# Gated attention and two FFNs: the first FFN's weight pieces through five staging buffers, high and low halves in slots of their own

## The reference

```python
state = f[:, :, t, :, None] * state + np.einsum('bhd,bhe->bhde', k[:, :, t], v[:, :, t])   # f = sigmoid(f_logit)
y[:, :, t] = np.einsum('bhd,bhde->bhe', q[:, :, t], state)
```

## Time and profile before

| | us |
|---|---|
| median of 3 runs (1322.17 to 1323.76) | 1322.76 |
| the profiled execution, its own time | 1321.92 |
| span of the profiled execution | 1320.1 |
| PE busy | 1306.3 |
| DVE (VectorE) busy | 832.0 |
| ACT busy | 623.1 |
| POOL (GpSimd) busy | 548.4 |
| PE's granted clock | 1.00 in every slice |

### The profile page before, as it was taken

How to read it: one execution, slowest core, us unless ns; L and a number is a source line. 1 busy time by engine, 2 the same in 40 slices (tenths; PEclk the granted TensorE clock), 3 DMA queues, 4 the chain that set the end, 5 groups by cost and what they waited for, 6 DMA issues and landing times.

```text
span 1320.1 us, 23658 instructions
## 1 busy us (share of the span) xinstructions
PE 1306.3 (99%) x8319; PEld 1282.8 (97%) x8319; DVE 832.0 (63%) x1678; ACT 623.1 (47%) x1259; POOL 548.4 (42%) x560
## 2 busy tenths in 40 slices
PE   8899999999999999999999999999999999999999
PEld 7889999999999999999999999999999999999998
DVE  7756455555543333357787677786767776777765
ACT  6544444544432223354445554455554456445441
POOL 4222121212117676144444654446644447444441
PEclk9999999999999999999999999999999999999999
DMA  7521212212113434123322243232343222343211
GB/s 219 170 72 51 59 48 66 59 48 66 44 34 96 136 104 131 65 79 89 93 88 79 90 132 94 89 97 72 97 132 89 86 79 84 103 132 94 89 59 49
DMA packets 71687, 117.61 MB, mean 89 GB/s; under 512 B 7120, under 2 KB 49808, under 8 KB 71568
## 3 DMA queue, kind: packets, MB, share of 16 engines
q1 hardware_dynamic: 71568, 116.08, 29.1%
HBM read 102.94 MB, written 14.55 MB: 89 GB/s over the span
## 4 chain that ended last, share of the span: by engine, by line
PE 96%; DVE 1%; issue 1%; ACT 1%; DMA 0%; SPq 0%; DVEq 0%; ACTq 0%
PE bank L1854 11%; PE bank L1856 11%; PE bank L1855 11%; PE bank L2075 10%; PE bank L2076 10%; PE bank L2077 10%; PE bank L1969 8%; PE bank L1971 8%; PE bank L1970 8%; PE bank L1798 2%; PE bank L1849 2%; PE bank L1837 1%; PE bank L2047 1%; PE bank L1781 1%; PE bank L2046 1%
## 5 line engine op out<-in xcount | busy, mean ns | idle before, releaser
L1241 POOL TENSOR_TENSOR wu<-w_r,wu 128x640 fp32r<-128x640 f32 (+1 forms) x132 | 201.1, 1526 | 314.3 <-ACT wu L927 314.3
L2075 PE MATMUL bank<-wd,h_hi 128*128 128x384 f32 x768 | 259.9, 338 | 0.5 <-issue 0.3
L2076 PE MATMUL bank<-wd,h_hi 128*128 128x384 f32 x768 | 257.5, 335 | 0.0
L2077 PE MATMUL bank<-wd,h_lo 128*128 128x384 f32 x768 | 257.1, 335 | 0.0
L1647 DVE SCALAR_TENSOR_TENSOR xt<-bank,pn,xt 128x384 f32<-128x384 f32 x288 | 177.2, 615 | 100.8 <-PE bank L2077 91.2
L954 ACT ACTIVATE h_hi<-h 128x384 fp32r<-128x384 f32 x240 | 124.7, 524 | 193.3 <-DVE h L1597 81.5
L1971 PE MATMUL bank<-x_lo,wu 128*128 128x384 f32 x600 | 202.5, 338 | 0.0
L1854 PE MATMUL bank<-xs_hi,wab 128*128 128x384 f32 x576 | 198.9, 345 | 2.9 <-DVE h_sb L1415 1.9
L1969 PE MATMUL bank<-x_hi,wu 128*128 128x384 f32 x600 | 201.4, 336 | 0.1
L1970 PE MATMUL bank<-x_hi,wu 128*128 128x384 f32 x600 | 200.8, 335 | 0.0
L1855 PE MATMUL bank<-xs_hi,wab 128*128 128x384 f32 x576 | 193.1, 335 | 0.0
(11 more groups left out here) (147 smaller groups left out, 2418.9 us busy)
## 6 DMA issues: line engine op xcount, KB each, us to landing
w_r<-weight_sums SPq DMA_DIRECT2D x120, 320.0 KB, 2.9
raw<-w SPq DMA_DIRECT2D x48, 576.0 KB, 3.9
unit<-fkq SPq DMA_DIRECT2D x28, 504.0 KB, 4.2
v_in<-v_chunks SPq DMA_DIRECT2D x32, 144.0 KB, 4.1
out<-xt SPq DMA_DIRECT2D x24, 192.0 KB, 4.0
weight_sums<-w_s SPq DMA_DIRECT2D x10, 384.0 KB, 4.4
weight_sums<-w SPq DMA_DIRECT2D x40, 64.0 KB, 2.7
raw<-wo SPq DMA_DIRECT2D x6, 384.0 KB, 3.4
```

The costliest lines, as they stand in the source:

```text
L1241: eng.tensor_tensor(wu_piece(g, n, 1), wu_raw(g, n), wu_piece(g, n, 0).bitcast(f32), ALU.subtract).then_inc(s_ulo, 1)
L2075: eng.matmul(o, hh, w_hi, start=(f == fs[0]), stop=False)
L2076: eng.matmul(o, hh, w_lo, start=False, stop=False)
L2077: mm = eng.matmul(o, hl, w_hi, start=False, stop=(f == fs[-1]))
```

## The change

Pieces 6 to 17 go through five places instead of two: the two of `raw` and the three of `raw_x`, which are free once pieces 0 to 2 are split. SP issues pieces 6 to 10 ahead of slot 0 and piece r + 5 one slot behind the low half of piece r. The high halves of pieces 6 and 7 and the low half of piece 6 are made ahead of slot 0; the others have slots of their own, `HI_AT` and `LO_AT`, the low half mostly a slot behind the high one, and in slots in which VectorE's FFN work of that slot (`h_rest` or `gate`) stands ahead of it. Unit 4's logs, sums and decays stand in slots 1, 2 and 3 instead of ahead of slot 0, in 1 and in 2. The hold on the last three pieces is split: the high half waits for the outputs and states of units 0 to 3, the low half for unit 4's output (piece 15) or unit 5's (16 and 17). Token tile 1 waits for the low half of piece 15 before it writes over `raw_x`. No computation is added or taken away.

```diff
--- before.py
+++ after.py
@@ -106,8 +106,10 @@
 
     LAST_OF_2 = dict(TOGETHER, state=5, output=7, y=8, store=9)
     LAST_OF_ALL = dict(TOGETHER, output=8, y=9, store=10)
+
+    FIRST_OF_2 = dict(CLOSE, logs=-7, sums=-6, decays=-5)
     UNIT_AT = {(step, J[u] + after): u for u in J
-               for step, after in (LAST_OF_2 if u == 2 * PPB - 1 else CLOSE if u < 2 * PPB else
+               for step, after in (FIRST_OF_2 if u == FIRST else LAST_OF_2 if u == 2 * PPB - 1 else CLOSE if u < 2 * PPB else
                                    LAST_OF_ALL if u == NU - 1 else TOGETHER).items()}
     CMIN_AT = J[NU - 1] + 8
     STRONG_AT = CMIN_AT + 9
@@ -139,7 +141,11 @@
     LOW_POOL = (0, 1, 2)
     LOW_DVE = (3, 4, 5)
 
-    SPLIT_AT = dict(zip((1, 3, 5, 7, 9, 10, 12, 14, 16, 19, 24, 29), range(EARLY, R1)))
+
+    RAWS = 5
+    AHEAD = 2
+    HI_AT = dict(zip((4, 6, 7, 9, 10, 12, 13, 18, 22, 25), range(EARLY + AHEAD, R1)))
+    LO_AT = dict(zip((4, 5, 7, 8, 10, 11, 13, 14, 19, 23, 26), range(EARLY + 1, R1)))
 
 
     SUMS_AT, SUMS_PACE = CMIN_AT, 8
@@ -296,7 +302,7 @@
         s_f = [sem(f"s_f{n}") for n in range(FIRST)]
         s_v = [sem(f"s_v{n}") for n in range(VRING)]
         s_early = [sem(f"s_early{n}") for n in range(EARLY)]
-        s_raw = [sem(f"s_raw{n}") for n in range(2)]
+        s_raw = [sem(f"s_raw{n}") for n in range(RAWS)]
         s_p = sem("s_p")
         s_set = sem("s_set")
         s_const = sem("s_const")
@@ -414,13 +420,14 @@
         def raw_place(r):
             if r < EARLY:
                 return (raw_x, raw_w)[r // (EARLY // 2)][:, r % (EARLY // 2), :]
-            return raw[:, r % 2, :]
+            n = (r - EARLY) % RAWS
+            return raw[:, n, :] if n < 2 else raw_x[:, n - 2, :]
 
         def raw_loaded(eng, r):
             if r < EARLY:
                 eng.wait_ge(s_early[r], 16)
             else:
-                eng.wait_ge(s_raw[r % 2], 16 * ((r - EARLY) // 2 + 1))
+                eng.wait_ge(s_raw[(r - EARLY) % RAWS], 16 * ((r - EARLY) // RAWS + 1))
 
         def split_done(eng, r):
             eng.wait_ge(s_whi, r + 1)
@@ -436,9 +443,16 @@
             eng.wait_ge(s_plo, len(LOW_POOL))
             eng.wait_ge(s_wlo, len(LOW_DVE))
 
-        def split_free(eng, r):
+
+
+        def hi_free(eng, r):
             if PIECES_1[r][0] == 2 and PIECES_1[r][2] * OPR >= FT1 // 2:
-                eng.wait_ge(s_y, OWN)
+                eng.wait_ge(s_y, FIRST)
+                eng.wait_ge(s_st, states(FIRST, 0))
+
+        def lo_free(eng, r):
+            if PIECES_1[r][0] == 2 and PIECES_1[r][2] * OPR >= FT1 // 2:
+                eng.wait_ge(s_y, OWN - 1 if (PIECES_1[r][2] + 1) * OPR <= FT1 // 2 + 3 else OWN)
 
 
         def x_tile(n, k):
@@ -457,7 +471,8 @@
             if n >= 2:
                 eng.wait_ge(s_upb, FT1 * (n - 1))
             else:
-                early_low_done(eng)
+
+                low_done(eng, EARLY + 2 * RAWS - 1)
 
 
         def group(g):
@@ -646,14 +661,18 @@
                    .then_inc(s_v[u % VRING], 16)
 
             def load_raw(r):
-                if r >= EARLY + 2:
-                    eng.wait_ge(s_whi, r - 1)
-                    low_done(eng, r - 2)
+                if r >= EARLY + RAWS:
+                    eng.wait_ge(s_whi, r - RAWS + 1)
+                    low_done(eng, r - RAWS)
+                elif r >= EARLY + 2:
+
+                    eng.wait_ge(s_whi, r - EARLY - 1)
+                    low_done(eng, r - EARLY - 2)
                 dst = raw_place(r)
                 src = pieces_1(r)[0]
                 if PIECES_1[r][0] == 2:
                     dst = dst.rearrange("p (j n) -> p j n", n=DM)
-                eng.dma_start(dst, src).then_inc(s_early[r] if r < EARLY else s_raw[r % 2], 16)
+                eng.dma_start(dst, src).then_inc(s_early[r] if r < EARLY else s_raw[(r - EARLY) % RAWS], 16)
 
 
             def load_w1(q):
@@ -748,8 +767,8 @@
             eng.dma_start(pn[:, :, :], probs).then_inc(s_p, 16)
             store_x(0)
             load_unit(FIRST + 1)
-            load_raw(EARLY)
-            load_raw(EARLY + 1)
+            for r in range(EARLY, EARLY + RAWS):
+                load_raw(r)
             for j in range(3 * N1):
                 if j == STRONG_AT:
                     flag = is_strong(eng)
@@ -759,8 +778,10 @@
                     load_unit(u)
                 if (u := at(j, "v")) is not None:
                     load_v(u)
-                if j - 1 in SPLIT_AT and SPLIT_AT[j - 1] + 2 < R1:
-                    load_raw(SPLIT_AT[j - 1] + 2)
+                if j == 1:
+                    load_raw(EARLY + RAWS)
+                if j - 1 in LO_AT and LO_AT[j - 1] + RAWS < R1:
+                    load_raw(LO_AT[j - 1] + RAWS)
                 if j == SUMS_AT - 3:
                     load_w1(0)
                 for q in range(NQ):
@@ -903,7 +924,7 @@
 
             def split_hi(r):
                 raw_loaded(eng, r)
-                split_free(eng, r)
+                hi_free(eng, r)
                 eng.activation(pieces_1(r)[1][0], loaded_1(r), ACT.Copy).then_inc(s_whi, 1)
 
             def x1_hi(n, k):
@@ -1003,7 +1024,8 @@
             x1_hi(0, 1)
             evac_y(3)
             x1_hi(0, 2)
-            logs(FIRST)
+            split_hi(EARLY)
+            split_hi(EARLY + 1)
             for j in range(3 * N1):
                 if j == STRONG_AT:
                     flag = is_strong(eng)
@@ -1025,8 +1047,8 @@
                     inverses(u)
                 if (u := at(j, "logs")) is not None:
                     logs(u)
-                if j in SPLIT_AT:
-                    split_hi(SPLIT_AT[j])
+                if j in HI_AT:
+                    split_hi(HI_AT[j])
                 for n in range(1, NB1):
                     for k in range(KT):
                         if x_at(n, k) == j:
@@ -1397,7 +1419,7 @@
                 eng.wait_ge(s_whi, r + 1)
                 if r == EARLY:
                     early_low_done(eng)
-                split_free(eng, r)
+                lo_free(eng, r)
                 hi, lo = pieces_1(r)[1]
                 eng.tensor_tensor(lo, loaded_1(r), hi.bitcast(f32), ALU.subtract).then_inc(s_wlo, 1)
 
@@ -1511,6 +1533,7 @@
             x_first_lo(2)
             first_lo(5)
             limit(FIRST)
+            first_lo(EARLY)
             for j in range(3 * N1):
                 if j == STRONG_AT:
                     flag = is_strong(eng)
@@ -1534,8 +1557,8 @@
                     sums(u)
                 if (u := at(j, "limit")) is not None:
                     limit(u)
-                if j in SPLIT_AT:
-                    first_lo(SPLIT_AT[j])
+                if j in LO_AT:
+                    first_lo(LO_AT[j])
                 for n in range(NXS):
                     if j == x2_at(n) - 1:
                         x2_sum(0, n)
```

## The result

The kernel after has a median of 1315.41 us (1314.87 to 1315.63) against 1322.76, five executions each; the ratio is 0.9943 with a 95% interval of 0.9929 to 0.9958. That is 7.35 us faster; 1316.3 had been forecast.

What follows compares the result with a forecast made beforehand. PE was taken to bound the kernel, with 8.07 us of waits to win; less 0.6, 0.9 and 0.1 that gave 6.5 us, 1316.3 us against the median of 1322.76. Range 1314.7 to 1319.3 us.

Steps and rivals of the forecast that it cites:

- What bounds it, and the most that it can give: Slots 0 to 30: PE bounds; its seven waits from 24 to 105 us, 6.95 + 7 x 0.16 = 8.07 us at most.
- The waits at 32.15 and 34.46: PE's waits of 0.97 us for `a_out(0)` and 0.48 us for `gate(0)`: gone, but for 0.06 of the first.
- `down_1(0)`: PE start at 37.50, wait 1.18 us: would start at 35.05, with 0.6 us remaining behind unit 4's chain.
- `down_1(1)`: PE start at 40.75 instead of the wanted 39.83, VectorE waiting out GpSimd's passes: 0.9 us remain, bounds 0 and 1.5.
- The reserve at `down_1(2)`: `h_rest(2)` ready at 45.4 where PE wants it at 45.73; margin 0.3 us, growing afterwards.
- the first rival: VectorE falls further behind: two more waits of 0.8 us at `down_1(2)` and (3), gain 4.9, 1317.9 us; chance 0.22.
- Starts 48.98 and 56.17: PE's waits of 1.55 and 0.48 us, from low halves of pieces 10 and 13 ahead of `h_rest(2)` and `h_rest(3)`: both gone.
- Starts 76.12 and 83.81: PE's waits of 1.45 us (old hold on piece 15) and 0.84 us (piece 16's low half ahead of `h_rest(7)`): both gone.
- The loads: Raw piece loads issued earlier on SP, each further piece 5 us or more ahead of its high half: cost 0.
- the crowd of loads: Rival: three more loads delay piece 7 by up to 3.8 us; gain 3.2 to 5, 1317.8 to 1319.6 us; chance 0.08.
- PE's idle time outside 25 to 100 us grows: Sign that the prediction is wrong: PE's idle time outside that span rising above 6.85 us.
- The slower rival: VectorE and GpSimd become the bound of slots 4 to 14: 7.8 us slower at worst, 1330.5 us; chance 0.03.

Runs made afterwards that it cites:

- front and hold: Kernel before with only the split hold, unit 4 in slots 1 to 3 and pieces 6 and 7 moved earlier; two places, other slots old: 1319.48 us, ratio 0.9973.

## Why the prediction was right

- **What bounds it, and the most that it can give.** Right: the gain lies in 25 to 100 us and is kept. The seven waits with 0.16 us each, 8.07 us, less what was left, gave 6.5; measured were 7.35 between medians and 6.3 between the profiled executions. By the prediction's own count, 8.07 less what is left, 0.76 + 2 x 0.16 = 1.08, the gain is 7.0 us; the terms put at 1.6 in sum were half a microsecond too high, and the rest of the difference is within the spread of the runs.
- **The waits at 32.15 and 34.46.** Gone as said; the second stood in the kernel before as

```profile
34.46 0.45 PE L1854 MATMUL bank<-xs_hi,wab 128*128 128x384 f32 x1 [0.48 <-DVE h_sb L1415]
```

  `a_out(0)` ran at 31.14, so 30.70 less the 0.44, the forecast value. Unit 4 moved alone took the first away and made the second 1.42 us; pieces 6 and 7 moved without unit 4 were not run.
- **`down_1(0)`.** 0.6 us were to remain; 0.18 of idle and 0.16 of the record, 0.34 remained. The chain behind it is the one named (logs, scans, decay pass, ends and limit).
- **`down_1(1)`.** 0.9 us were to remain, at 40.75; it started at 40.77, or 40.33 less the 0.44, with 0.53 + 0.16 = 0.7 us. The cause was shown by the short GpSimd passes. But the size is in part luck, for the step to it had the order wrong: I let VectorE and GpSimd take turns and so had piece 7's low half wait ("near 1.9"). It took 0.95; VectorE went on from `h_rest(0)` to piece 7 without a gap and GpSimd's first pass waited through both (1.98), then the keys, which need that pass and meet the second one, took 1.37. The Trainium skill's page SBUF — State Buffer, section Who interferes with whom, says that the later of the two is kept out; the runs agree (0.55 against 1.37 with the passes cut to 16 columns) and add that the next VectorE instruction can go ahead of a GpSimd pass that was there first (piece 7's low half at 35.10, the pass at 34.96).
- **The reserve at `down_1(2)`**, said to be 0.3 us and the place of the first rival. It was mis-sized for that same reason: `h_rest(2)` was to be ready at 45.4 and was at 44.08, less 0.44 43.6, 1.8 us earlier. Ahead of it VectorE lost only some 0.4 us, on a copy (0.60, where unit 4's took 0.17), and GpSimd paid (2.56); the keys' 1.38 came behind it. PE came to it at 45.84, so the reserve was 1.8 us. The first rival had no ground.
- **Starts 48.98 and 56.17.** Gone as said, with one misreading: the low half ahead of `h_rest(3)` was piece 12's, in slot 12 (53.53, 1.20 us in the trace of before), not piece 13's, which stood behind it in slot 14; and `h_rest(3)` was itself held, 1.37 us for 0.55. The runs name both conditions: new slots (2.8 us of idle time between front and hold and the kernel after) and the order inside the slot (2.9 us).
- **Starts 76.12 and 83.81.** The hold explains the first, as said. The second was put down to piece 16's slot; that step failed. With the hold alone and piece 16 in its old slot the wait went too, so both belong to the one stall, 2.29 us of idle time. With the new hold the new slots of pieces 15 to 17 were not needed: with front and hold, the last three in their old slots, no wait was left behind 55.66.
- **The loads.** "Cost 0" was right for PE. Piece 7's load came 0.22 us late for ACT (30.13), all that the crowd of loads did. A wait of ACT for a load there was named as a sign of being wrong; this one stood ahead of nothing late, as `a_out(0)` behind it still waited 0.17 us for PE. What I did not say is that the five places are not needed at all with these slots. The sign "PE's idle time outside 25 to 100 us grows" came true to the letter (7.4 for 6.85 us) and misled: 0.42 of it is in the first 25 us, where the profiles differ by more than that.
- The slower rival had no trace of itself. What can make this front slower was shown elsewhere: unit 4's chain moved without the halves, 5 us.

## What to carry to other kernels

When a bound engine waits a few tenths here and there, read what stands ahead of the late instruction in its own engine's list: here that order, and one wait that was stricter than the data needed, were the whole 7 us, and buffers and earlier loads alone were worth nothing. Test the parts of such a change apart, since one of them made the kernel slower alone, and compare idle times only between profiles with the same granted clock, since a slow clock hid a wait of 0.92 us. A stall on a helper engine can cost more than its own wait (2.29 us for 1.45 here), since the slots behind it meet no reserve; take away the longest first and look again.

## What the runs showed that was not expected

- PE's clock is at stake in short waits: 3.52 us without work were followed by a granted clock of 0.51 over 3 us and cost 1.6 us more; 1.89 us by 0.83 and 0.71 in one profile, by 1.00 in another with the same wait. In the first of these PE took 0.3 us longer to `down_1(3)`, as the slow matmuls took the place of a wait.
- VectorE's scans are held by GpSimd's passes too: three took 2.66 us instead of 1.05. So are copies of 112 x 3 numbers (0.60 us instead of 0.17).
- Where VectorE has its next instruction ready, a GpSimd pass of 1.02 us can wait through two or three of them (1.98 and 2.56 us). Not always: the next in the second case, the keys at 44.00, had to wait for the pass (1.38 us).
